# Attention in 32-partition blocks: VectorE block transposes, 32-column products and ranks from one-hots

## The reference, cut

```python
def sm_attn(qq, kk, vv):              # softmax(qq kk^T / 8) vv
    ...
p_packed = sm_attn(p, k, v)           # p: 32 packed queries per head
x = sm_attn(q, p_packed, p_packed)    # 8 batches, 8 heads, 576 tokens, 64 wide
x = x.transpose(0, 2, 1, 3).reshape(4608, 512)
expert = argmax(x @ w_gate); y = gate * relu(x @ w1[expert]) @ w2[expert]   # 8 experts, 1024 wide
out = (s * relu(y @ w_in) ** 2 + b) @ w_out                                 # 2048 wide
```

## Time and profile before

| | before |
|---|---|
| time, median of 3 runs | 1612.56 us (1609.71 to 1615.33) |
| the profiled execution | 1613.26 us, of which span 1611.5 us |
| PE busy, share of the span | 1507.4 us, 94% |
| DVE, ACT, POOL busy | 457.5, 471.7, 458.3 us |
| bytes moved | 126.22 MB |

### The profile page before, as it was taken

The page is one execution under the profiler, slowest core; times in us unless marked ns, Lnnn a source line. Parts: engine busy times, 40 slices in busy tenths (PEclk is TensorE's granted clock), DMA queues, the critical chain, the costliest instruction groups (busy, mean ns, idle before and its releaser), DMA issues.

```text
span 1611.5 us, 24870 instructions
## 1 busy us (share of the span) xinstructions
PE 1507.4 (94%) x8930; PEld 1228.6 (76%) x8931; DVE 457.5 (28%) x720; ACT 471.7 (29%) x823; POOL 458.3 (28%) x393
## 2 busy tenths in 40 slices
PE   6988808999999999997799999999999999999998
PEld 5877706888888888886588888888888888888886
DVE  2556631111111111111433223232323223232322
ACT  3555402222222222221222223222322223222222
POOL 1066669663753873601900000000000000000000
PEclk6889858999999999999799999999999999999999
DMA  9889545432433432411300001010100000000000
GB/s 239 198 238 249 147 154 142 147 104 85 143 97 92 150 117 78 137 41 36 120 20 33 14 14 39 7 39 13 39 7 33 20 13 33 12 33 0 26 0 27
DMA packets 96911, 126.22 MB, mean 78 GB/s; under 512 B 50656, under 2 KB 69088, under 8 KB 95712
## 3 DMA queue, kind: packets, MB, share of 16 engines
q1 hardware_dynamic: 41696, 84.44, 17.9%
q10 hardware_dynamic: 49216, 21.05, 4.9%
q0 software_dynamic: 5952, 20.06, 4.1%
HBM read 90.76 MB, written 34.77 MB: 78 GB/s over the span
## 4 chain that ended last, share of the span: by engine, by line
PE 91%; POOL 3%; issue 2%; DMA 2%; DVE 1%; ACT 1%; SPq 0%; ACTq 0%; POOLq 0%; DVEq 0%
PE psum L679 18%; PE psum L681 18%; PE psum L680 18%; PE psum L759 8%; PE psum L761 8%; PE psum L760 8%; PE psum L581 2%; PE psum L723 2%; PE psum L534 1%; PE psum L747 1%; PE psum L619 1%; PE psum L688 1%; POOL x_by_expert L426 1%; PE psum L600 1%; PE psum L569 1%
## 5 line engine op out<-in xcount | busy, mean ns | idle before, releaser
L1194 DVE SCALAR_TENSOR_TENSOR s_r_r<-r_relu,s_col 128x512 f32<-128x512 f32 x144 | 113.6, 789 | 456.4 <-ACT r_relu L968 456.4
L679 PE MATMUL psum<-weights_split,gT_hi 128*128 128x512 f32 x576 | 231.2, 401 | 3.4 <-DVE gT_lo L1196 3.4
L759 PE MATMUL psum<-yT_hi,weights_split 128*128 128x512 f32 x576 | 228.5, 397 | 1.4 <-issue 1.4
L384 POOL TENSOR_TENSOR weights_split<-weights_raw,one 128x1024 fp32r<-128x1024 f32 x80 | 153.0, 1912 | 268.1 <-PE psum L681 237.8
L760 PE MATMUL psum<-yT_lo,weights_split 128*128 128x512 f32 x576 | 228.6, 397 | 0.0
L761 PE MATMUL psum<-yT_hi,weights_split 128*128 128x512 f32 x576 | 228.6, 397 | 0.0
L681 PE MATMUL psum<-weights_split,gT_lo 128*128 128x512 f32 x576 | 228.6, 397 | 0.0
L680 PE MATMUL psum<-weights_split,gT_hi 128*128 128x512 f32 x576 | 228.3, 396 | 0.0
L968 ACT ACTIVATE r_relu<-psum 128x512 f32<-128x512 f32 x144 | 86.2, 598 | 467.9 <-PE psum L761 467.9
L469 POOL DMA_INDIRECT y_gathered<-y_by_slot,tpos x36 | 34.5, 960 | 583.9 <-PE psum L747 581.9
L386 POOL TENSOR_TENSOR weights_split<-weights_raw,weights_split 128x1024 fp32r<-128x1024 f32 x80 | 192.7, 2409 | 6.3
(11 more groups left out here) (154 smaller groups left out, 1854.1 us busy)
## 6 DMA issues: line engine op xcount, KB each, us to landing
weights_raw<-in_moe_w_dram SPq DMA_DIRECT2D x64, 512.0 KB, 3.6
x_slot<-x_by_expert ACTq DMA_DIRECT2D x40, 256.0 KB, 3.2
y_by_slot<-y_slot ACTq DMA_DIRECT2D x40, 256.0 KB, 2.1
k_sb<-in_k_dram SPq DMA_DIRECT2D x16, 576.0 KB, 7.0
q_sb<-in_q_dram SPq DMA_DIRECT2D x16, 576.0 KB, 7.9
v_sb<-in_v_dram SPq DMA_DIRECT2D x16, 576.0 KB, 5.2
out_dram<-out_sb SPq DMA_DIRECT2D x9, 1024.0 KB, 3.9
weights_raw<-in_moe_w_in_dram SPq DMA_DIRECT2D x8, 512.0 KB, 3.1
```

What stands on the lines that cost most here:

```text
L384: nc.gpsimd.tensor_tensor(hi, raw[c_ % 2][:], one[:].to_broadcast([P, CH]), ALU.mult).then_inc(hi_done, 1)
L679: nc.tensor.matmul(dst, lhs[0][:, col:col + P], rhs[0], start=first_, stop=False)
L759: nc.tensor.matmul(ps[:, HFB + f % 2, :], w[0], yT[0][:, k_, :], start=(k_ == 0), stop=False)
L1194: nc.vector.scalar_tensor_tensor(sq[par][:], rel[:], s_col[:], rel[:], ALU.mult, ALU.mult).then_inc(sq_done, 1)
```

## The change

A head's 576 tokens now lie on 32 partitions, 18 tokens (4608 B) each, and the 4 heads fill 128 partitions. K and Q take 18 transposes of 128x128 per unit (`turn_k`, `turn_kq`, `turn_q`). Both probability matrices are turned by DVE in 32x32 blocks instead of by TensorE and ACT. The products with them are therefore cut to 32 rows or 32 columns: 72 products each in `score_packs`, `mix_packs` and `mix_values`, where there were 12, 24 and 24. `mix_values` gives its result transposed, per half of the array, and `sum_values` adds the halves and turns it back. Expert logits go to a tile of their own (`out_logits`), so that scattered rows are 2048 B. Token ranks come from TensorE products of the one-hots (`ranks`, `positions`); `count` and GpSimd's arithmetic in `scatter` are gone. In the attention stage ACT rounds the weights' high part and GpSimd the low. The loads of s and b, the 1.8 MB of zeros for unused slot rows and the `el`/gate steps move to later places; the P load comes first.

```diff
-                return src[b, qd * HQ:(qd + 1) * HQ].rearrange("h (p j) d -> p h (j d)", p=SP_)
+                return src[b, qd * HQ:(qd + 1) * HQ].rearrange("h (p j) d -> (h p) (j d)", p=NPK)
...
             def score_packs(u):
-                pe.wait_ge(bd_done, u + 1)
-                pe.wait_ge(qa_done, u + 1)
-                pe.wait_ge(qb_done, min(u + 2, UNITS))
+                pe.wait_ge(pkt_done, u + 1)
+                pe.wait_ge(t2_done, u + 1)
                 passed()
-                for t in range(CJ):
+                for t in range(TT):
+                    at = 2 * TT - 6 + t if t < 6 else TT + t - 6
                     for h in range(HQ):
-                        dst = s2_ps[:, 2 * t:2 * t + 2, h, :]
-                        last = nc.tensor.matmul(dst, qT[u % 2][:, h, t * SP_:(t + 1) * SP_], bd[:, h, :], start=True, stop=True)
+                        for par in range(2):
+                            half, cols = slice(par * D, (par + 1) * D), slice(h * NPK, (h + 1) * NPK)
+                            last = nc.tensor.matmul(ps[cols, S2_AT + par, t * NPK:(t + 1) * NPK], kqT[u % 2][half, at, cols], pkT[half, cols],
+                                                    start=True, stop=True)
...
             def mix_packs(u):
+                pe.wait_ge(exp1_done, min(u + 3, UNITS))
...
+                for t3 in range(TT // 3):
+                    for par in range(2):
+                        for c in range(3):
+                            for h in range(HQ):
+                                heads, j = slice(h * NPK, (h + 1) * NPK), 2 * t3 + par
+                                last = nc.tensor.matmul(ps[c * NPK:(c + 1) * NPK, X_AT + h, j * XS:j * XS + XC], a2T[heads, par, 3 * c + t3, :],
+                                                        pkx[u % 2][heads, D:D + XC], start=True, stop=True)
...
+                for t in range(TT):
+                    for par in range(2):
                         for h in range(HQ):
+                            heads, half = slice(h * NPK, (h + 1) * NPK), slice(par * D, (par + 1) * D)
+                            last = nc.tensor.matmul(ps[half, PV_AT + h, 0:NPK], v_sb[u % 2][heads, 2 * t + par, :], a1T[heads, par, t, :],
+                                                    start=(t == 0), stop=(t == TT - 1))
+                last.then_inc(pv_full, 1)
+
+            def sum_values(u):
+                pe.wait_ge(pv_done, u + 1)
+                passed()
+                for h in range(HQ):
+                    last = nc.tensor.matmul(ps[h * NPK:(h + 1) * NPK, PK_AT, 0:D], pvT[:, h, :], halves[:], start=True, stop=True)
...
+            def turn_keys(u):
+                dve.wait_ge(exp1_done, u + 1)
+                need(dve, pv_full, u)
+                nc.vector.transpose(a1T[:].rearrange("p a t n -> p (a t n)"), a1[:].rearrange("p a n -> p (a n)")).then_inc(a1t_done, 1)
```

More of the change, by code:

```diff
@@ L16 @@
 NPK = 32
+E = 8
 SP_ = 96
@@ L437, in _ @@
                     scatter(b - 1)
[L438 to L440 removed]
+                round_low(b, b, 0)
             scatter(B - 1)
@@ L544, in turn_qa, with turn, turn_k @@
-            def turn_qa(u):
-                need(pe, xb_done, u - 2)
-                turn_q(u, 0, QA, qa_full)
+            def turn(bank, blocks, full):
+                for i, (rows_, t) in enumerate(blocks):
+                    last = nc.tensor.transpose(ps[:, bank + i // 3, (i % 3) * P:(i % 3 + 1) * P], rows_[:, t * P:(t + 1) * P], ident[:])
+                last.then_inc(full, 1)
+            def turn_k(u):
+                need(pe, pv_done, u)
+                pe.wait_ge(k_in[u % 2], 16 * (u // 2 + 1))
+                turn(T0_AT, [(k_sb[u % 2], t) for t in range(6)], t0_full)
@@ L586, in score_packs, with ranks @@
                 last.then_inc(gate_full, 1)
-            def cursors(b):
-                pe.wait_ge(cnt_ready, b + 1)
+            def ranks(b):
+                pe.wait_ge(oh_done, b + 1)
+                need(pe, rank_read, b)
                 passed()
-                nc.tensor.matmul(ps[0:SP_, PKB, CUR_AT:CUR_AT + E], ones[:], cum[:], start=True, stop=False)
-                nc.tensor.matmul(ps[0:SP_, PKB, CUR_AT:CUR_AT + E], lower[:], cnt[:], start=False, stop=True).then_inc(cur_full, 1)
@@ L595, in turn_a1 @@
-            def turn_a1(u):
-                pe.wait_ge(exp1_done, u + 1)
-                for i in range(2):
-                    for t in range(CJ):
-                        last = nc.tensor.transpose(ps[0:SP_, MID + i, t * P:(t + 1) * P], a1[:, i, t * SP_:(t + 1) * SP_], ident[:])
-                last.then_inc(a1t_full, 1)
+                dst = ps[0:SP_, RANK_AT, 0:(J + 1) * E]
+                oh_ = oh[b % 2]
+                nc.tensor.matmul(dst, ident[0:SP_, 0:SP_], base[:].unsqueeze(1).to_broadcast([SP_, J + 1, E]), start=True, stop=False)
@@ L603, in mix_packs @@
+                nc.tensor.matmul(dst[:, 0:J * E], lower[:], oh_[:].rearrange("p j e -> p (j e)"), start=False, stop=False)
+                for j in range(J):
+                    last = nc.tensor.matmul(dst[:, (j + 1) * E:], ones[:], oh_[:, j, :].unsqueeze(1).to_broadcast([SP_, J - j, E]),
+                                            start=False, stop=(j == J - 1))
+                last.then_inc(rank_full, 1)
             def mix_packs(u):
@@ L1107, in _ @@
+                if it >= 3 and it % 2 == 1:
+                    experts((it - 3) // 2)
+            positions(B - 1)
             done = [0]
```

570 lines of the change are left out of this document (259 added, 311 removed).

## The result

The changed kernel takes 1710.2 us (median of 4 runs, 1702.75 to 1711.92) beside 1613.4 us for the kernel before on the same chip: a ratio of 1.061 (95% interval 1.058 to 1.064), 97 us slower. The profiled execution took 1708.86 us, span 1707.1.

A forecast was written before the change was run, and what follows sets the result against it. TensorE's instruction supply was taken to bound the units: 1611.5 + 159 (fifteen units) - 8 (first blocks) - 4 (start) - 10 (tail) = 1748.5 us of span, about 1750 us; range 1565 to 1785 us.

The forecast's parts named there:

- starved of instructions: Attention units: TensorE waits for its next instructions, 21.5 us a unit, about 1750 us in all; chance 0.45.
- both main signs: Whole kernel: slower, chance 0.63, or faster, chance 0.34.
- middle rival: Units: small products cost a floor each or blocks come in half the time; 14.5 us a unit, 1652 us; chance 0.18.
- units of 20 us or more: Attention units: one of the signs that would show TensorE starved of instructions.
- The mechanism: Units: "issue" as TensorE's largest idle releaser, about 60 instruction packets before the routing, DVE and ACT under half busy.
- 21.5 us a unit: Units: 966 instructions at 21 to 25 ns; each unit 10.6 us longer, fifteen of them 159 us.
- the 8 forecast: First units: the first instruction blocks are there at the start, 8 us less.
- TensorE's own 9.2 us: Units: TensorE's work with instructions always at hand, 9.2 us a unit from 10.9, bounds 7.6 to 15.7.
- The start: Before the first `score_keys`: b moves away and P lands first, 4 us less (0 to 6).
- The last units: Behind the fifteen units: the last two iterations hold some 860 instructions, 19 us, as long as now.
- The tail: Last `out_x` to landed scatter: 24 us for 33.9, 10 us less; zero rows can give back up to 7.
- The block transpose: VectorE in the units: priced as a copy of 128x576, 0.758 us, from 0.6 to twice that.

The follow-up runs named there:

- e5: e4 with the ten middle units of TensorE's program as a loop of five rounds of two units: 1637.7 us.
- e4: Changed kernel, unrolled, with `mix_packs` as 24 products of 96 columns of weights a unit in place of 72 of 32: 1675.5 us.
- e2: Kernel before with 300 nearly empty products more a unit, all on one tile of the array: 1807.8 us.
- e8: Kernel before with P loaded first and the loads of s and b moved behind the first expert's chunks: ratio 1.000.
- e12: e8 with TensorE's wait for the gate weights moved from ahead of the first key transposes to ahead of the first `score_packs`: ratio 1.000 against the kernel before.
- e11: Changed kernel with the zero rows of y written at unit 4 in place of behind the routing: 1752.4 us, on a slower chip.
- e9: e5 with `score_packs` as 24 products of 96 columns of data and the zero rows of y written early: 1646.7 us, ratio 0.999 against the kernel before.
- e7: Kernel before with 300 nearly empty products more a unit, taken in turn on three tiles of the array: 1748.8 us.
- e6: Changed kernel, unrolled, with `mix_packs` and `score_packs` in 24 products each and `mix_values` in 36: 1628.9 us, ratio 1.009 against the kernel before.

## Why the prediction was right, and where it was not

The likeliest case, starved of instructions, came true, 40 us short of its number, and below its own range of 1725 to 1790. The recorded range, 1565 to 1785 us, was drawn to hold both main signs and would have held a faster kernel as well, and 1710.2 is also the top of the middle rival's 1600 to 1710. So the time alone doesn't choose the case; the waits, the packets and e5 do. One sign failed (units of 20 us or more; they took 17.96, the full ones 18.69).

- **The mechanism.** The prediction read it from three waits of 6.4 us in all. After, "issue" on the three groups is TensorE's largest wait, as forecast, the units moved 54 packets (forecast some 60), and DVE and ACT are under half busy. e5 against e4 shows it as the cause: the same products, with their instructions kept in the engine, take 9.8 us a unit where fetched ones take 17.4. The middle rival's signs are absent: the product groups cost 16 ns a pass, not above 20, TensorE was idle 31% of the units, and two packets came in 10.0 us, not 7.5.
- **The term that was off: 21.5 us a unit.** A full unit took 18.69, 19.2 ns an instruction, where the prediction took 21 to 25 from the earlier trace rows. Over fifteen units that is 42 us too much, and the shorter first ones give 3 more than the 8 forecast. Two packets came in 10.0 us, where the earlier trace rows have 10.5 to 12.7 for about as many: a rate read from stretches in which TensorE rarely waited was not the rate of the supply. Nor is there one rate: the full units of e4 took 16.68 us and 21.3 ns an instruction (10172 in 216.80 us). Its 192 instructions fewer saved 2.0 us, 10 ns each and not 19, so the unit is not simply its instructions times a rate. What law it follows stays open.
- **TensorE's own 9.2 us.** At full clock it was near. In e5 from 112.75 to 131.69 us, at a granted clock of 1.00, `score_packs` and `mix_values` took 7.2 us for 576 passes, 12.5 ns each (priced at 12):

```profile
L562 PE MATMUL psum<-pkT,kqT 64*32 64x32 f32 x288 | 3.9, 200 | 0.2
L623 PE MATMUL psum<-a1T,v_sb 32*64 32x32 f32 x288 | 3.3, 225 | 0.0
```

 In the changed kernel it was 12.4 us busy at 0.61. The prediction took the low clock to be hidden under starvation. e4 and e5 show that about half of the gap is busy time at the low clock.
- **Two rules of the Trainium skill.** That the cost of fetching is mostly hidden (Runtime: NRT & Kernel Launch, Instruction fetch mechanics) didn't hold, as the prediction said. Nor did some 60 cycles for each matmul (TensorEngine Tiling (Array Packing), Instruction Overhead), 25 ns at the high clock: a pass took 11.5 to 13.5 ns here on 8 parts of the array. Even in a row on one tile a product took 28.5 ns at a mean clock of 0.61 (e2), where 60 cycles would be 41.
- **The start: -5.5, forecast -4 (0 to 6),** with a wrong reason. b was the last of three small loads behind one wait; e8 moved it and won nothing. What helps is that the wait for the gate weights no longer holds up the transposes: 2.8 us in e12. Of the 3.0 us that the changed kernel is still ahead of e12, 1.7 lie before the first key transpose (9.35 us by the timeline, in e12 11.05; P lands 1.0 us earlier) and 1.3 between it and `score_keys` (2.8 us, in e12 4.1), where the changed kernel turns in 18 transposes what e12 turns in 24. Neither was tried by itself.
- **The last units: +9.9, forecast 0.** The stretch from the sixteenth `score_keys` on holds three iterations, not two: 1829 recorded matmuls and loads, a full unit more than the 860 that I had counted. The fifteen units of the sum are the distances between sixteen starts, and the sixteenth unit was left out. A full unit got 8.1 us longer (18.69 against 10.62, the thirteen full ones of before), which is most of the 9.9.
- **The tail: -12.3 to the landed scatter, forecast -10; +4.2 behind it, forecast up to 7 given back** to the zeros. The size was right. e11 clears the zeros of y alone; the zero rows of x (`x_by_expert<-zeros`, L335) stay where they are in it, and the load of the first expert rows waits for them as well as for the scatter. Their last was issued at 235.6 us before and at 336.9 after; the load followed at 240.42 and 340.57, which is 1.98 and 4.05 us behind the landed scatter. It then took 3.4 us to land before and 4.9 after, with the DMA engines at 0.44 and 0.91. These two make 3.6 of the 4.2 us. The first, 2.1 us, is what the prediction had in mind, but by the rows of x and not of y. All of this is read from the traces, and no run moved the rows of x.

 `el` and the work that needs it also moved behind the landing. In the changed kernel VectorE is done with it before ACT releases `xT_lo`; in e11 it holds `xT_lo` up. Rows of before, after and e11:

```profile
240.42 0.70 ACTq L889 DMA_DIRECT2D x_slot<-x_by_expert  x1
```
```profile
346.57 0.20 DVE L1144 TENSOR_TENSOR slot_row_of_token_sb<-row_of_token_sb,pos_s 96x48 int32<-96x48 int32 x1
347.74 0.69 DVE L1149 TENSOR_TENSOR xT_lo<-psum,xT_hi 128x512 fp32r<-128x512 f32 x1 [0.96 <-ACT xT_hi L845]
```
```profile
391.61 0.69 DVE L1151 TENSOR_TENSOR xT_lo<-psum,xT_hi 128x512 fp32r<-128x512 f32 x1 [0.96 <-DVE slot_row_of_token_sb L1146]
```

 The 6.7 us won behind the first expert product were not forecast. TensorE's wait for split weights is 1.3 us there and was 3.4; the cause of the rest is open.
- **The block transpose:** 0.77 us, priced at 0.758.

## What to carry to other kernels

Count TensorE's instructions for each stretch, not only its products: an unrolled stretch with little work in each of them can wait for its own program, and a few unexplained "issue" waits before a change that multiplies instructions are the sign. Look whether the waits stand one packet's worth of instructions apart; small ones in a stretch without packets (e9) are something else. Then ask whether a round can be a loop short enough to stay in the engine (here 1548 matmuls and loads did, but for one return of four, and 1932 didn't), or whether wider products really cost less array time. When a sum multiplies by the number of units, check how many of them the stretch holds. And when one small load is taken away from ahead of a wait, look at which load behind the same wait lands next.

## What the runs showed that I had not expected

- A loop's round can stay resident for 31.7 us and 2687 matmuls and loads without one packet of instructions (e5), and can also be fetched again in the middle.
- Small products on one tile cost 28.5 ns, the same ones on three tiles in turn 11.6 ns (e2, e7; clocks 0.61 and 0.54).
- A TensorE that was busy 98% with such products was granted 0.61 in the mean (e2). In e5 it was granted 1.00 from 112.75 to 131.69 us, busy 89% with small products and without packets, and 0.51 in the unit that was fetched again.
- Three units of e9 took 19 us at 0.60 to 0.66, two of them without a packet of instructions.
- 24 products with 32 rows and 96 columns of weights take 1.3 us a unit (e6, 17.4 us for 624 passes), while 36 with 128 columns take 3.0, both at a mean clock of 0.80.
- A load of 16 KB behind those of P, K, Q and V takes 9.55 us to land (e8).
